# First MLP's work dealt in halves beside attention; P\*V in the transposes' PSUM bank

## The reference

```python
# q, k, v: [4, 8, 576, 64]; tau = 0.02
scores = (q @ k.T) / 8
thresh = max(scores, -1) - tau
scores = where(scores >= thresh, scores, -1e9); scores -= max(scores, -1)
attn = exp(scores); attn /= sum(attn, -1) + 1e-9
x = (attn @ v)                       # as [2304 tokens, 512]
h = x @ w_in1;  x2 = (h * sigmoid(1.702 h)) @ w_out1     # 512 -> 2048 -> 512
h = x2 @ w_in2; out = (h * tanh(softplus(h))) @ w_out2
```

## Time and profile before

| what | value |
|---|---|
| median of 3 runs | 1185.55 us (1183.62 to 1186.87) |
| profiled execution | 1183.23 us, its span 1180.6 us |
| PE busy | 1097.8 us (93%) |
| DVE, ACT, POOL busy | 788.9, 732.0, 336.4 us |
| mean granted clock of PE | 0.978 |

### The profile page before, as it was taken

One profiled execution on the slowest core, in us unless ns is written; L12 is line 12 of the kernel. 1 busy time (PEld: TensorE's weight loads), 2 busy tenths in 40 slices (PEclk: granted clock), 3 DMA queues, 4 the chain that ended last, 5 costly groups with the idle time before them and its releaser, 6 DMA issues.

```text
span 1180.6 us, 19607 instructions
## 1 busy us (share of the span) xinstructions
PE 1097.8 (93%) x7472; PEld 1046.3 (89%) x7472; DVE 788.9 (67%) x1404; ACT 732.0 (62%) x1008; POOL 336.4 (28%) x654
## 2 busy tenths in 40 slices
PE   5667998899998999999999999999999999999998
PEld 4557898899998999999989999998998989899897
DVE  5887897688887988888888633576334444443343
ACT  5667876677777877778767522367456544654453
POOL 6866554344444544455444100000000000000000
PEclk9777999999999999999999999999999999999999
DMA  8632223223223323233232001630000000001000
GB/s 252 199 81 85 55 64 104 58 75 101 56 79 108 75 76 93 62 87 92 79 102 54 22 30 56 214 98 27 1 27 27 28 27 27 27 17 38 1 27 27
DMA packets 95117, 81.48 MB, mean 69 GB/s; under 512 B 47664, under 2 KB 80432, under 8 KB 95024
## 3 DMA queue, kind: packets, MB, share of 16 engines
q1 hardware_dynamic: 95024, 80.24, 23.4%
HBM read 66.06 MB, written 14.16 MB: 68 GB/s over the span
## 4 chain that ended last, share of the span: by engine, by line
PE 81%; DVE 11%; ACT 3%; issue 3%; POOL 1%; DMA 0%; SPq 0%; ACTq 0%; DVEq 0%; POOLq 0%
PE ps_s L679 17%; PE ps_r L574 16%; PE ps_r L595 13%; PE ps_r L702 9%; PE ps_r L465 7%; PE ps_t L449 5%; PE ps_s L437 5%; PE ps_t L702 4%; PE ps_t L595 3%; DVE e_buf L505 2%; DVE pt_lo L518 2%; DVE neg_max L497 1%; PE ps_t L574 1%; DVE q_st L396 1%; DVE x_lo L735 1%
## 5 line engine op out<-in xcount | busy, mean ns | idle before, releaser
L746 DVE COPY hidden<-ps_s 128x768 f32<-128x768 f32 x48 | 45.9, 957 | 170.5 <-PE ps_s L679 170.5
L574 PE MATMUL ps_r<-x_hi,wi_lo 128*128 128x256 f32 x544 | 158.5, 291 | 0.0
L574 PE MATMUL ps_r<-x_lo,wi_hi 128*128 128x256 f32 x544 | 154.2, 283 | 0.0
L574 PE MATMUL ps_r<-x_hi,wi_hi 128*128 128x256 f32 x544 | 154.1, 283 | 0.0
L449 PE MATMUL ps_t<-ident,e_buf 128*128 128x128 f32 x720 | 108.9, 285 | 35.1 <-DVE pt_lo L518 33.1
L775 ACT ACTIVATE m_lo_raw<-m_lo_raw 128x1536 f32<-128x1536 f32 x24 | 35.8, 1491 | 168.8 <-DVE m_lo_raw L753 168.8
L595 PE MATMUL ps_r<-g_hi,wo_lo 128*128 128x256 f32 x464 | 135.8, 293 | 3.7 <-DVE g_lo L624 3.5
L518 DVE TENSOR_TENSOR pt_lo<-ps_t,pt_hi 128x640 fp32r<-128x640 f32 x144 | 118.1, 820 | 31.5 <-ACT pt_hi L485 29.9
L485 ACT CAST pt_hi<-ps_t 128x640 fp32r<-128x640 f32 x144 | 100.0, 694 | 59.3 <-PE ps_t L449 55.7
L595 PE MATMUL ps_r<-g_hi,wo_hi 128*128 128x256 f32 x464 | 131.6, 284 | 0.0
L595 PE MATMUL ps_r<-g_lo,wo_hi 128*128 128x256 f32 x464 | 131.5, 283 | 0.0
(11 more groups left out here) (96 smaller groups left out, 3107.5 us busy)
## 6 DMA issues: line engine op xcount, KB each, us to landing
k_ll_raw<-in_k SPq DMA_DIRECT2D x64, 288.0 KB, 2.8
v_st_raw<-in_v SPq DMA_DIRECT2D x64, 160.0 KB, 3.0
wi_lo_raw<-in_moe_w_in SPq DMA_DIRECT2D x16, 512.0 KB, 4.4
wo_lo_raw<-in_moe_w_out SPq DMA_DIRECT2D x16, 512.0 KB, 5.7
q_raw<-in_q SPq DMA_DIRECT2D x32, 192.0 KB, 2.9
x_lo_raw<-x_scratch SPq DMA_DIRECT2D x9, 512.0 KB, 4.2
x_scratch<-y_acc SPq DMA_DIRECT2D x9, 512.0 KB, 3.5
x_lo_raw<-x_scratch SPq DMA_DIRECT2D x6, 768.0 KB, 4.7
```

The lines of the kernel that those rows point to most:

```text
L574: mm = pe.matmul(bank[:, part * CH:(part + 1) * CH], wi[w][:, k, f * P:(f + 1) * P], x[:, k, :], start=t == 0, stop=t == 3 * KT - 1)
```

## The change

Pieces are dealt in halves (`HALVES_AT`): each step from 21 on takes one or two halves, spread evenly, with a chunk's first no earlier than `READY`; the total beside attention stays 108 pieces. Step by step: steps 21 to 42 hold the 32 halves of chunk 0 (formerly steps 23 to 40); of the 56 steps with P\*V of groups 8 to 63 the last has no transposes and so no wait for the sum, 40 have two halves and 16 one; of the other 70 steps from 21 on 20 have one half and 50 two. No step has none. A down starts at least two steps behind the up that it needs.

The first 8 groups (the first 256 tokens) are no longer stored and loaded: DVE adds P\*V straight into `x_raw`.

From group 8 on P\*V goes to columns 128 to 447 of `ps_t`'s second bank, behind the fifth turned tile; the ring of `ps_r` is for pieces alone. In those steps PE does P\*V, transposes 0 to 3, scores, waits for DVE's sum of P\*V, then the fifth transpose and then all of the step's halves. ACT normalises n-1 before it takes the high part of n-2; DVE sums P\*V before the row maximum.

Weights are loaded one piece a step in steps 0 to 15 and split in the order and steps given.

```diff
-READY = [GROUPS[g][4] + 8 for g in CHUNK_GROUP]
+READY = [GROUPS[g][4] + (6 if c == 0 else 8) for c, g in enumerate(CHUNK_GROUP)]
-for k in range(BESIDE):
-    slot = max(slot, READY[0] + k * (N + 3 - READY[0]) // BESIDE)
-    ...
-    PIECES_AT[slot].append(k)
+for n in range(READY[0], N + 3):
+    if n < READY[1]:
+        behind = (n + 1 - READY[0]) * FIRST_CHUNK // (READY[1] - READY[0]) - done
+    else:
+        behind = FIRST_CHUNK + (n + 1 - READY[1]) * (2 * BESIDE - FIRST_CHUNK) // (N + 3 - READY[1]) - done
+    for _ in range(min(behind, 2)):
+        ...
+        HALVES_AT[n].append((PIECES[k], part))
...
         def x1_stores(g):
+            if g < H:
+                return []
...
+        def pv_bank(g):
+            return ps_r[:, g % 2, 0:320] if g < H else ps_t[:, 1, P:P + 320]
...
-        W_SLOT = {4 + 2 * c: c for c in range(2 * PAIRS)}
+        W_ORDER = [0, 1, 2, 3, 8, 9, 4, 5, 10, 11, 6, 7, 12, 13, 14, 15]
+        W_SLOT = dict(zip((6, 9, 12, 14, 16, 18, 20, 22, 24, 26, 27, 28, 30, 31, 33, 34), W_ORDER))
...
         def pe_pv(pe, g):
-            ring_release(pe, ("pv", g))
+            if g >= 2:
+                pe.wait_ge(s["pv_sum"], g - 1 if g < H else g)
...
         def act_x_hi(act, c):
-            act.wait_ge(s["x_in"], 16 * (c + 1))
+            if c == 0:
+                act.wait_ge(s["pv_sum"], H)
+            else:
+                act.wait_ge(s["x_in"], 16 * c)
...
 +                pe_pv(pe, g)
                 if n - 2 < N:
-                    pe_turn(pe, n - 2)
+                    pe_turn(pe, n - 2, range(NJ - 1))
                 if n + 1 < N:
                     pe_scores(pe, n + 1)
-                for piece, part in todo[len(todo) // 2:]:
+                if n - 2 < N:
+                    pe.wait_ge(s["pv_sum"], g + 1)
+                    pe_turn(pe, n - 2, range(NJ - 1, NJ))
+                for piece, part in halves:
                     pe_half(pe, piece, part)
...
 +                if FRONT <= n - 1 < N:
+                    act_norm(act, n - 1)
                 if not turn_first and 0 <= n - 2 < N:
                     act_p_hi(act, n - 2)
-                if FRONT <= n - 1 < N:
-                    act_norm(act, n - 1)
...
 +                if n >= FRONT + 2 and n - 3 in GROUP_AT:
+                    dve_pv(dve, GROUP_AT[n - 3])
                 if 0 <= n < N:
                     dve_max(dve, n)
...
-                if n >= FRONT + 2 and n - 3 in GROUP_AT:
-                    dve_pv(dve, GROUP_AT[n - 3])
...
 -                if n < 8:
-                    w_load(sp, 0, 2 * n)
-                    w_load(sp, 0, 2 * n + 1)
+                if n < 2 * PAIRS:
+                    w_load(sp, 0, W_ORDER[n])
```

More of the change, by code:

```diff
@@ L110 @@
     CHUNK_GROUP.append(need)
-READY = [GROUPS[g][4] + 8 for g in CHUNK_GROUP]
+READY = [GROUPS[g][4] + (6 if c == 0 else 8) for c, g in enumerate(CHUNK_GROUP)]
+HALVES_AT = [[] for _ in range(N + 3)]
 PIECES_AT = [[] for _ in range(N + 3)]
+START_SLOT = {}
+TAKEN = {}
+FIRST_CHUNK = 2 * PIECES.index(("up", PAIRS))
 BESIDE = PIECES.index(("down", QUARTERS * (CHUNKS - 3) + 2, 0))
-slot = 0
-for k in range(BESIDE):
-    slot = max(slot, READY[0] + k * (N + 3 - READY[0]) // BESIDE)
-    if PIECES[k][0] == "up" and PIECES[k][1] % PAIRS == 0:
-        slot = max(slot, READY[PIECES[k][1] // PAIRS])
-    PIECES_AT[slot].append(k)
[L120 to L128, removed]
+done = 0
+for n in range(READY[0], N + 3):
[4 more added lines that the diff above has]
+    for _ in range(min(behind, 2)):
+        k, part = done // 2, done % 2
+        if PIECES[k][0] == "down" and PIECES[k][2] == 0 and part == 0:
+            if n < TAKEN[2 * PIECES[k][1] + 1] + 2:
+                break
+        if PIECES[k][0] == "up" and PIECES[k][1] % PAIRS == 0 and part == 0:
+            if n < READY[PIECES[k][1] // PAIRS]:
+                break
+            START_SLOT[PIECES[k][1] // PAIRS] = n
+        HALVES_AT[n].append((PIECES[k], part))
+        if part == 1:
+            PIECES_AT[n].append(k)
+            if PIECES[k][0] == "up":
+                TAKEN[PIECES[k][1]] = n
+        done += 1
+assert done == 2 * BESIDE
+ALONE = range(BESIDE, len(PIECES))
 CH2 = 384
@@ L439, in pe_scores, with pe_turn @@
             mm.then_inc(s["qk_done"], 1)
[L441 to L448, removed]
+        def pe_turn(pe, n, tiles=range(NJ)):
+            if 0 in tiles:
+                if n < FRONT:
+                    pe.wait_ge(s["normed_first"], n + 1)
+                else:
+                    pe.wait_ge(s["normed"], n - FRONT + 1)
+                if n >= 1:
+                    pe.wait_ge(s["p_lo"], n)
+            for j in tiles:
                 mm = pe.transpose(t_flat[:, j * P:(j + 1) * P], e_buf[n % 3][:, j * P:(j + 1) * P], ident[:, :])
-            mm.then_inc(s["turned"], 1)
+            if NJ - 1 in tiles:
+                mm.then_inc(s["turned"], 1)
         def pe_pv(pe, g):
             _, _, _, u, last = GROUPS[g]
-            bank = ring_bank(("pv", g))
             pe.wait_ge(s["p_lo"], last + 1)
@@ L520, in dve_pv @@
         def dve_pv(dve, g):
-            base = (GROUPS[g][1] % 2) * D
+            h = GROUPS[g][1]
+            base = (h % 2) * D
             w = group_cols(g)[1]
             par, grp = x1_place(g)
-            c = grp * 256
             dve.wait_ge(s["pv_half"], g + 1)
[L526 to L529, removed]
+            if g < H:
+                rows = x_raw[base:base + D, h // 2, 0:w]
+            else:
+                rows = x_pair[base:base + D, grp * 256:grp * 256 + w]
+                if x1_count(g, (par, grp)):
+                    dve.wait_ge(x1_out[par][grp], 16 * x1_count(g, (par, grp)))
+            dve.tensor_tensor(rows, pv_bank(g)[0:D, 0:w], pv_half_sb[base:base + D, 0:w], ALU.add).then_inc(
+                s["pv_sum"], 1)
         def pool_row(pool, n):
@@ L658, in sp_y_store @@
             sp.dma_start(x2_dram[:, :, c * CH:(c + 1) * CH], y_acc[:, :, :]).then_inc(s["y_out"], 16)
-        X_HI = {START_SLOT[c] - 2: c for c in range(CHUNKS) if START_SLOT[c] is not None}
+        X_HI = {slot - 2: c for c, slot in START_SLOT.items()}
         def pe_up2(pe, g):
@@ L1069, in _ @@
                 for c in range(CHUNKS):
-                    if START_SLOT[c] is not None and START_SLOT[c] - 4 == n:
+                    if c >= 1 and START_SLOT.get(c) == n + 4:
                         sp_x_load(sp, c, stores)
```

90 lines of the change are left out of this document (45 added, 45 removed).

## The result

The changed kernel takes **1175.98 us** (median of 5 runs, 1171.59 to 1176.98) against 1185.55 (1183.01 to 1186.87) for the kernel before in the same rounds: a ratio of **0.9922, 95% interval [0.9902, 0.9942]**, a gain of 9.6 us. A second set of runs gave 1174.79 us and 0.9913 [0.9898, 0.9929]. The profiled execution took 1176.4 us, its span 1174.6, 6.0 less than before.

What follows compares the result with a forecast made beforehand. PE bounds from step 21 on, with 38.5 us of holes; before that DVE. 1183.2 - 38.5 - 3 - 3 + 16 + 8 + 6 + 3.5 + 2 = 1174.2, plus 2.3: 1176.5 us, range 1159 to 1195.

Steps and rivals of the forecast that it cites:

- Holes and thin steps: From step 21 on: PE's holes go, -38.5 us; thin steps +8 and +6, chunk starts +3.5, moved weight splits +2.
- The wait for P\*V: Before the fifth transpose, from group 8 on: 55 new PE waits of 0.21 or 0.31 us, 14.7, plus 1.7 restarting: +16.
- Clock: From 94.8 to 208.2 us: halves instead of holes take back 3 of the 4.5 us lost to the lower clock.
- First stage: Before step 21: seven instead of nine weight pieces split, and one load a step, together -3 us.
- the two moved splits: Two weight splits reappear behind step 21, where DVE has about 4.05 us per step and PE 4.12: +2 us.
- Rival C: Steps 21 to 43: if DVE is the bound, halves in the holes only push its work; 1183.5 us, no change; chance 0.15.
- Median over the profiled execution: Whole kernel: the median of the runs was 2.3 us above the profiled execution, so 2.3 was added at the end.
- A: Whole kernel: DVE and ACT keep up everywhere, thin steps cost nothing, only the wait's floor counts; 1155.5 us; chance 0.20.
- B: PV steps: ACT and DVE are locked to PE, P*V's sum 0.4 us late in each of 55 steps; 1199 us; chance 0.20.
- (1): Before the fifth transpose: PE's waits for DVE x_pair appear 40 to 56 times, mean 0.2 to 0.4 us.
- (5): PE's clock is about 0.99 from 100 to 200 us.
- (7): PE's idle time from step 21 to the last P*V is about 36 us, where it was 38.5.

Runs made afterwards that it cites:

- experiment 2: Changed kernel, but ACT copies half of P*V twice in groups 8 to 63, first to a spare tile: 1188.16 us, 1.0028 to the kernel before.
- experiment 4: Changed kernel with pieces dealt whole from step 21 on, P*V still in the fifth tile's bank: 1220.84 us, 1.0311 to the kernel before.
- Experiments 3: Changed kernel with P*V back in the two ring banks and the former order in PV steps, halves still dealt: 1254.88 us, 1.0588 to the kernel before.
- Experiment 5: Changed kernel with the former order, steps and loads of the weights: 1176.88 us, 0.9932 to the kernel before.
- experiment 8: Changed kernel with its first piece at step 23 again, all else kept: 1176.89 us, 0.9928 to the kernel before.
- experiment 6: Changed kernel with the low parts of ten weight pieces (steps 20 to 34) moved from DVE to POOL: 1174.54 us, 0.9909 to the kernel before.
- experiment 9: Changed kernel, but from group 8 on DVE and ACT copy P*V's halves side by side and POOL adds them: 1173.05 us, 0.9900 to the kernel before.

## Why the prediction was right, and where it wasn't

1176.5 us was forecast, 1175.98 measured. Its terms against its own base of the profiled execution come to 1174.2; that execution took 1176.4. The trace bears out the mechanism and most of the sizes, but the terms are not all right:

- **Holes and thin steps** (-38.5, +8, +6, +3.5, +2: net -19.0). Measured net -6.8 - 10.5 - 4.0 + 1.1 = **-20.2**. The sum is right: start to start, holes of 44.0 us stood there before and 23.7 are left, where the busy view had 38.5 and the thin steps were put at 19.5. By kind of step, from step 44 on (excess over PE's work, small gaps included): a PV step with one half 0.85 us in 12 cases, with two 0.47 in 33; another step with one half 0.44 in 11, with two 0.12 in 46. The half more or less costs 0.38 and 0.32, where 0.5 and 0.3 stood, but a step with two halves isn't free.
- **The wait for P\*V** (14.7 in 55 waits, 1.7 for starting again: 16). Measured 13.8 in 53, and 4.4 where 1.7 stood: **18.2**, or 19.0 with the wait of step 144, whose missing scores the sum had overlooked. The total is right by two errors: the chain with both engines ready costs 0.11 and 0.23 where 0.21 and 0.31 stood (PE goes on 0.05 to 0.06 behind DVE's end, where the prediction allowed up to 0.15), and ten late sums make up for it. The 0.03 read from the earlier trace rows was the restart of transposes; the change from transposes to the next matmul, 0.08, was missed. 
- **Clock** (-3). Nothing came: 6.0 us lost before and 5.9 after. The step failed in this: it took the clock of steps 21 to 43 as the price of their long waits, which the halves would remove. Some are left. In the changed kernel's trace the clock fell to the half twice after 97 us, at 137.6 and 161.5 us. Just before each PE had two holes, of 1.3 and 0.8 us, from start to start (ending at 135.9 and 137.3, and at 159.7 and 161.0). The same two pairs of holes stand in the second profile of the same program, where only the second was followed by a fall, and in experiment 2's, where neither was. In steps 21 to 43 half of the time on the lower clock, which is the most that it can cost, was 5.8 and 3.7 us in the changed kernel's two profiles and between 1.6 and 6.0 in the experiments (12.6 in experiment 4). In the kernel before, the falls at 104.8, 196.9 and 217.4 us stood beside holes of 1.7, 2.8 and 3.7 us, while one of 2.7 that ended at 368.9 brought none. So such holes can cost the clock and need not; what decides it these runs don't say. Experiments 3 and 4, with longer holes, spent 58 and 56 us on the lower clock.
- **First stage** (-3). Measured -2.8 in this trace, -4.4 in the second profile (90.38 us). Experiment 5 has step 21 begin at 95.8 without the new order, so the term is there; the same experiment shows that little of it reaches the end. The +2 that stood for the two moved splits is neither confirmed nor ruled out.
- **Steps 21 to 43.** Rival C, at 0.15, was right there: halves in the holes gave nothing (+1.3 for equal work), and experiment 8 found 2 us at most in the early start. Its cause isn't borne out: taking 10 splits off DVE (experiment 6) didn't mend it. What bounds these steps stays open; the excess of a step there is 0.75 to 1.37 us against 0.12 to 0.85 later, with no one wait that carries it.
- **Median over the profiled execution** (+2.3). Before, the profiled execution was 2.3 under the median; after, it was 0.4 over it. These 2.7 us hid the 2.2 by which the sum of the terms was too low. The hit within 1 us is partly luck; the sum is good to about 3.

The rivals: **A** (only the floor, 1155.5) is out; thin steps do cost, and even without the wait for P\*V the kernel takes 1163.75. **B** (1199) is out: its lateness is there in ten steps, not in 55, and DVE mostly idles before the sum rather than being late for it. Experiment 2, which lengthens the chain by 0.27 in each PV step, shows what less than B's 0.4 already does: 1188, the gain gone, as its break-even of 0.16 a step asks.

The signs: (1) wrong as asked, the view shows 10 waits for x_pair, not 40 to 56; from start to start there are 53 of mean 0.26, as said. (2) Right, from step 21 on the longest wait for pt_lo is 1.6. (3) Right. (4) Right, 91.98. (5) Wrong, 0.96. (6) Right, 98 us. (7) 36 us of idle were forecast; in the view of busy time it is 8.9 + 14.0 = 22.9, since it hides the short waits; from start to start, holes and the wait come to 17.2 + 2.1 + 0.3 + 4.1 + 13.8 = 37.5. DVE was busy 84% of 208.2 to 665 us, under the 92% that would have spoken against the prediction.

## What to carry to other kernels

When an engine that bounds has holes, small parts of independent work dealt into every step fill them only if each part has a buffer that is free then; give the third user of a ring of two a place outside it, even at the price of a short wait. Price such a wait by its chain (last matmul, copy, sum, hand-over) less the work that PE can do before it, and test it from both sides, by removing it and by lengthening its chain. Beside a DVE that is 85% busy, half or more of a wait removed can come back as another. Count short waits, and what an added instruction costs, from start to start, not by idle time or shown length.

## What the runs showed of the chip that I had not expected

- **Overlapping lengths hide waits.** The waits before the fifth transpose, 55 of 14.6 us in all, are shown as 10 waits of 5.1 us in the whole trace:

```profile
PE ps_t L460 <- DVE x_pair L544: 5.1, 10, 0.9
```

- **ACT's shown lengths overlap too.** A copy of 0.37 us held the next one back by 0.27 (experiment 2).
- **The granted clock of the first 100 us differs between executions of the same program.** In slices of 20 us the changed kernel had 0.88, 0.69, 0.73, 0.58 from 20 to 100 us, and in its second profile

```profile
20.00:40.00 20.00, 14.71 (x81) 12.90 (x80) 18.02 (x43) 12.02 (x21) 15.58 (x29) 0.83 0.68 204
40.00:60.00 20.00, 13.26 (x66) 11.56 (x64) 16.70 (x36) 14.15 (x24) 14.80 (x27) 0.74 0.74 223
60.00:80.00 20.00, 13.71 (x73) 12.80 (x74) 16.93 (x38) 11.42 (x20) 11.75 (x21) 0.76 0.42 130
80.00:100.00 20.00, 13.35 (x72) 11.54 (x72) 15.96 (x33) 15.74 (x25) 12.98 (x23) 0.72 0.18 46
```

  (the column before the last two). Step 21's P\*V started at 91.98 and 90.38 us. A term of 1 or 2 us in such a stretch can't be read from one profile.
- **A DVE subtraction with both inputs in SBUF and a POOL addition wait for each other**: 1.20 us instead of 0.68 for DVE and 1.24 instead of 0.74 for POOL (experiment 9). Work moved to an idle POOL wasn't free.
